# A fused attention, Fourier and channel-mixing kernel: the order of SyncE's transfers in the lead-in, two waits in the channel products, and what ScalarE and VectorE do for the turning angles

## The reference

```python
for t in range(S):
    ar, ai = (a_re_n[:, :, t, :, None], a_im_n[:, :, t, :, None])
    new_re = ar * S_re - ai * S_im
    new_im = ar * S_im + ai * S_re
    kv = np.einsum('bhd,bhe->bhde', k[:, :, t], v[:, :, t])
    S_re, S_im = (new_re + kv, new_im)
    y[:, :, t] = np.einsum('bhd,bhde->bhe', q[:, :, t], S_re)
```

## Time and profile before

| what | us |
|---|---|
| three runs | 1108.66, 1102.98, 1101.28; median 1102.98 |
| the profiled execution: its own time | 1107.81 |
| its span, first to last instruction | 1105.8 |
| TensorE busy, and mean granted clock | 1018.0 and 0.951 of full speed |
| VectorE, ScalarE, GpSimd busy | 533.7, 339.8, 16.3 |

### The profile page before, as it was taken

How to read it: one execution, slowest core, us unless ns; L and a number is a source line. 1 busy time by engine, 2 the same in 40 slices (tenths; PEclk the granted TensorE clock), 3 DMA queues, 4 the chain that set the end, 5 groups by cost and what they waited for, 6 DMA issues and landing times.

```text
span 1105.8 us, 15696 instructions
## 1 busy us (share of the span) xinstructions
PE 1018.0 (92%) x6154; PEld 975.5 (88%) x6154; DVE 533.7 (48%) x1046; ACT 339.8 (31%) x514; POOL 16.3 (1%) x12
## 2 busy tenths in 40 slices
PE   0469699989989999999999999998999999999997
PEld 0358589979979988999999999998999999999997
DVE  6797958998982555432423322542224223322321
ACT  7635545654721141122112211423112121220210
POOL 0000000000000000000000000021000000000000
PEclk9869869989978899999999999998999999999999
DMA  4559776876558106402102020001001001000000
GB/s 154 151 147 310 214 219 170 264 219 183 167 148 289 47 21 248 139 21 66 43 28 71 28 85 16 8 22 43 22 8 57 21 0 64 14 7 21 8 16 23
DMA packets 96602, 104.67 MB, mean 95 GB/s; under 512 B 13089, under 2 KB 90145, under 8 KB 96546
## 3 DMA queue, kind: packets, MB, share of 16 engines
q1 hardware_dynamic: 96546, 103.94, 30.4%
HBM read 70.80 MB, written 33.11 MB: 94 GB/s over the span
## 4 chain that ended last, share of the span: by engine, by line
PE 74%; DVE 14%; DMA 4%; issue 3%; SPq 1%; ACT 1%; POOL 1%; POOLq 0%; DVEq 0%; ACTq 0%
PE bank L232 20%; PE bank L234 19%; PE bank L233 19%; PE bank L1132 3%; PE bank L1193 2%; DVE n_area L906 2%; PE bank L1148 2%; DMA q_turn<-n_area 2%; PE bank L1209 1%; PE bank L1150 1%; PE bank L1161 1%; DVE x_flat L858 1%; PE bank L1211 1%; PE bank L242 1%; DVE n_area L911 1%
## 5 line engine op out<-in xcount | busy, mean ns | idle before, releaser
L120 ACT ACTIVATE hh<-bank 128x384 fp32r<-128x384 f32 x192 | 94.5, 493 | 386.4 <-PE bank L234 382.7
L208 DVE SCALAR_TENSOR_TENSOR hl<-bank,hh 128x384 fp32r<-128x384 f32 x192 | 107.0, 558 | 205.0 <-ACT hh L120 205.0
L232 PE MATMUL bank<-nTh,w1h 128*128 128x384 f32 x576 | 194.3, 337 | 6.1 <-DVE hl L208 3.6
L234 PE MATMUL bank<-nTh,w1l 128*128 128x384 f32 x576 | 193.6, 336 | 0.0
L233 PE MATMUL bank<-nTl,w1h 128*128 128x384 f32 x576 | 193.5, 336 | 0.0
L232 PE MATMUL bank<-w2h,hh 128*128 128x384 f32 x576 | 193.2, 335 | 0.0
L234 PE MATMUL bank<-w2h,hl 128*128 128x384 f32 x576 | 192.5, 334 | 0.0
L233 PE MATMUL bank<-w2l,hh 128*128 128x384 f32 x576 | 192.4, 334 | 0.0
L232 PEld LDWEIGHTS bank<-nTh,w1h 128*128 128x128 f32 x576 | 109.1, 189 | 7.1 <-DVE hl L208 3.9
L233 PEld LDWEIGHTS bank<-nTl,w1h 128*128 128x128 f32 x576 | 109.1, 189 | 0.0
L234 PEld LDWEIGHTS bank<-nTh,w1l 128*128 128x128 f32 x576 | 109.0, 189 | 0.0
(11 more groups left out here) (155 smaller groups left out, 1286.2 us busy)
## 6 DMA issues: line engine op xcount, KB each, us to landing
w_area<-k_turn SPq DMA_DIRECT2D x24, 384.0 KB, 3.5
w_area<-q_turn SPq DMA_DIRECT2D x24, 384.0 KB, 4.4
q_turn<-w_raw SPq DMA_DIRECT2D x30, 192.0 KB, 4.3
k_turn<-n_area SPq DMA_DIRECT2D x24, 192.0 KB, 4.0
k_turn<-w_flat SPq DMA_DIRECT2D x24, 192.0 KB, 4.6
u_scratch<-h_area SPq DMA_DIRECT2D x24, 192.0 KB, 2.9
w_raw<-in_moe_w_ch SPq DMA_DIRECT2D x2, 2304.0 KB, 12.1
x_flat<-u_scratch SPq DMA_DIRECT2D x4, 1152.0 KB, 9.8
```

The source lines that it names most:

```text
L120: self.nc.scalar.activation(self.hh[:, m, :], self.mm_bank[(g * (KF + TPG) + m) % 2][:, 0:TG], ACT.Relu).then_inc(self.h_high, 1)
L208: self.nc.vector.scalar_tensor_tensor(out=self.hl[:, m, :], in0=self.mm_bank[(g * (KF + TPG) + m) % 2][:, 0:TG], scalar=0.0, in1=self.hh[: ...
L232: self.nc.tensor.matmul(out, lh, rh, start=(n == 0), stop=False)
L234: last = self.nc.tensor.matmul(out, ll, rh, start=False, stop=(n == len(pairs) - 1))
```

## The change

On SyncE: `turn_over` is cut into `turn_out` (the writes) and `turn_back` (the reads), and `turn_decay` into `decay_out` and `decay_back`. For a part's first two blocks both writes come before both reads. `decay_out` is issued a step before `decay_back`. The q and k of p0 go to free columns of the other buffer, so the load of p2's q and k waits for nothing and is issued ahead of all turning. The later loads of gates and of q and k come one step earlier. On VectorE: L879 and L897 go; ScalarE makes the same number by `Sign` and `Identity` into `t4`, behind `Arctan`. `ends` keeps only its copy, and one reduce over all parts' `dstage` replaces L868 and L871. `products` treats two blocks with one instruction each (L922, L923, L925, L926 on 768 elements), and `products(p0)` moves ahead of `phases(p1)`. In the channel products, the wait of L1280 moves behind the first `hidden`, and that of L828 behind the first `high_hidden`.

```diff
...
+                self.qs, self.q0 = (1, 2 * CT) if n == 0 else (n % 2, 0)
...
-        GA = 14
-        GV = [12 + 5 * p.chunks for p in parts]
+        PAIRS = [[range(i, min(i + 2, p.chunks)) for i in range(0, p.chunks, 2)] for p in parts]
+        GA = 16
+        GV = [10 + 3 * p.chunks + 2 * len(PAIRS[p.n]) for p in parts]
...
             def load_qk(p):
-                if p.turn:
-                    before = parts[p.n - 2]
+                if p.n == 3:
+                    sp.wait_ge(k_out[0], 32)
+                    sp.wait_ge(q_out[0], 32)
+                if p.n > 2:
                     sp.wait_ge(vec_step[p.s], vec0[p.n])
...
-            turn_over(0)
-            turn_decay(p0)
+            load_qk(p2)
+            decay_out(p0)
+            decay_out(p1)
+            turn_out(0)
+            decay_back(p0)
+            decay_back(p1)
+            turn_back(0)
+            turn_out(1)
+            turn_out(2)
             load_gates(p3)
-            load_qk(p2)
-            turn_over(1)
-            turn_over(2)
-            turn_decay(p1)
+            turn_back(1)
+            turn_back(2)
             for m in range(NM):
                 if (m - 1, 4) in stage_at:
-                    p = stage_at[m - 1, 4]
-                    turn_over(p.first)
-                    turn_over(p.first + 1)
+                    first = stage_at[m - 1, 4].first
+                    turn_out(first)
+                    turn_out(first + 1)
+                    turn_back(first)
+                    turn_back(first + 1)
                 if (m - 1, 5) in stage_at:
-                    turn_over(stage_at[m - 1, 5].first + 2)
+                    last = stage_at[m - 1, 5].first + 2
+                    turn_out(last)
+                    turn_back(last)
+                if (m, 3) in stage_at:
+                    decay_out(stage_at[m, 3])
                 if (m, 4) in stage_at:
-                    turn_decay(stage_at[m, 4])
+                    decay_back(stage_at[m, 4])
                 for n, i in added_at(m - 1):
                     store_u(n, i)
-                if m % 3 == 1:
-                    for p in parts[2:]:
-                        if p.n > 3 and p.first == m + 8:
-                            load_gates(p)
-                        if p.n > 2 and p.first == m + 5:
-                            load_qk(p)
-                        if p.first == m + 2:
-                            load_v(p)
+                for p in parts[2:]:
+                    if p.n > 3 and p.first == m + 9:
+                        load_gates(p)
+                    if p.n > 2 and p.first == m + 6:
+                        load_qk(p)
+                    if p.first == m + 2:
+                        load_v(p)
...
                 A(t3_b[s][:, :, T], t3_b[s][:, :, T], ACT.Arctan).then_inc(act_step[s], 1)
+                A(im_b[p.r][:, :, T], re_b[p.r][:, :, T], ACT.Sign, scale=3.0,
+                  bias=nearly_zero[:, 0:1]).then_inc(act_step[s], 1)
+                act.wait_ge(act_step[s], act0[p.n] + 12)
+                A(t4[:, :, angles_room(p)], im_b[p.r][:, :, T], ACT.Identity, scale=-0.25,
+                  bias=quarter[:, 0:1]).then_inc(act_step[s], 1)
...
-            act.wait_ge(s1.w2_split, 3)
             with act.Fori(0, B - 1) as b:
                 s1.high_hidden(act, b, 0)
+                act.wait_ge(s1.w2_split, 3)
...
-                V.tensor_copy(dstage[:, s, :, 0:p.chunks], t2_b[s][:, :, CT - 1:p.T:CT]).then_inc(vec_step[s], 1)
-                dve.wait_ge(vec_step[s], vec0[p.n] + 5)
-                V.tensor_reduce(least_now[:, :], dstage[:, s, :, 0:p.chunks], mybir.AxisListType.XY,
-                                ALU.min).then_inc(least_step, 1)
-                dve.wait_ge(least_step, 2 * p.n + 1)
-                V.tensor_tensor(least[:, :], least[:, :], least_now[:, :], ALU.min).then_inc(least_step, 1)
+                V.tensor_copy(dstage[:, p.n, :, 0:p.chunks], t2_b[s][:, :, CT - 1:p.T:CT]).then_inc(vec_step[s], 1)
...
-                V.tensor_scalar(im[:, :, T], re[:, :, T], 0.0, -2.0 / PI, ALU.is_lt, ALU.mult).then_inc(vec_step[s], 1)
...
-                dve.wait_ge(act_step[s], act0[p.n] + 11)
-                dve.wait_ge(vec_step[s], n + 7)
-                V.scalar_tensor_tensor(out=t3_b[s][:, :, T], in0=im[:, :, T], scalar=1.0 / PI, in1=t3_b[s][:, :, T],
-                                       op0=ALU.add, op1=ALU.mult).then_inc(vec_step[s], 1)
-                dve.wait_ge(vec_step[s], n + 10)
-                V.tensor_scalar(im[:, :, T], re[:, :, T], 0.0, 0.5, ALU.is_lt, ALU.mult).then_inc(vec_step[s], 1)
+                dve.wait_ge(act_step[s], act0[p.n] + 13)
+                V.scalar_tensor_tensor(out=t3_b[s][:, :, T], in0=t3_b[s][:, :, T], scalar=1.0 / PI, in1=im[:, :, T],
+                                       op0=ALU.mult, op1=ALU.mult).then_inc(vec_step[s], 1)
...
-                for i in chunks:
-                    T = slice(i * CT, (i + 1) * CT)
+                for pair in chunks:
+                    i = pair.start
+                    T = slice(i * CT, pair.stop * CT)
...
+            products(p0, PAIRS[0])
             phases(p1)
-            products(p0, range(1))
             squared(p2)
-            products(p1, range(2))
+            products(p1, PAIRS[1])
...
+            V.tensor_reduce(least[:, :], dstage[:, :, :, :], mybir.AxisListType.XYZ, ALU.min).then_inc(least_found, 1)
...
-            pe.wait_ge(s0.w2_split, KF // 2)
             with pe.Fori(0, B - 1) as b:
                 s0.hidden(pe, b, 0)
+                pe.wait_ge(s0.w2_split, KF // 2)
                 s0.output(pe, b, 0)
...
```

More of the change, by code:

```diff
@@ L396, in forward @@
         a_mid = in_late(1, FH)
-        dstage = in_late(P, 2, 3, 3)
+        dstage = in_late(P, len(parts), 3, 3)
         YR = 12
@@ L490, in load_qk @@
             def load_qk(p):
-                if p.turn:
-                    before = parts[p.n - 2]
+                if p.n == 3:
+                    sp.wait_ge(k_out[0], 32)
+                    sp.wait_ge(q_out[0], 32)
+                if p.n > 2:
                     sp.wait_ge(vec_step[p.s], vec0[p.n])
-                    for m in range(before.first, before.end):
+                    for m in range(parts[p.n - 2].first, parts[p.n - 2].end):
                         sp.wait_ge(k_out[m % RING], 32 * (m // RING + 1))
                 for dst, src in ((k_b, lay["k"]), (q_b, lay["q"])):
-                    sp.dma_start(dst[p.s][:, :, 0:p.T], src[p.b, :, :, p.t0:p.t0 + p.T]).then_inc(qk_in[p.s], 16)
+                    sp.dma_start(dst[p.qs][:, :, p.qk_cols(0, p.chunks)],
+                                 src[p.b, :, :, p.t0:p.t0 + p.T]).then_inc(qk_in[p.s] if p.n else qk_first_in, 16)
             def load_v(p):
@@ L525, in turn_over, with decay_out @@
                 sp.dma_start(qT[:, r, :, :], back("q_turn")).then_inc(q_back[r], 16)
-            def turn_decay(p):
+            def decay_out(p):
                 if p.turn:
@@ L988, in _ @@
             squared(p1)
[L989 removed]
+            dve.wait_ge(consts_set, 5)
             logs(p0)
```

86 lines of the change are left out of this document (49 added, 37 removed).

## The result

The changed kernel takes 1059.13 us, median of 4 runs (1050.0 to 1066.06); the kernel before took 1102.47, median of 4 (1101.28 to 1108.66). The ratio is 0.9584, with a 95% interval of 0.9494 to 0.9675: 4.2% faster. The ratio is taken from the fast runs alone, without the one of 1066.06, so it isn't the quotient of the two medians, 0.9607. I had said 1058, within 1040 to 1084. The profiled execution after took 1054.72 us, with a span of 1052.7; the one before took 1107.81, with a span of 1105.8.

A forecast was written before the change was run, and what follows sets the result against it. TensorE was taken to bound the kernel throughout, losing time to waits and low clock. The terms summed to 47.1 us off the profiled 1107.8, so 1060.7, or 1055.9 from the median; the middle, 1058, was forecast, range 1040 to 1084.

The forecast's parts named there:

- lead-in: Start of the kernel, up to TensorE's step 1: mask multiply 0 comes earlier, p2's q no longer waited for; 4.7 us.
- step 21: TensorE's step 21 in the first half, low clock without a wait before it: no gain in the sum.
- Step 6: TensorE's wait for block 6's keys goes, 8.8 us, and the low clock behind it, 8.4 us.
- rival 3: Transfers collide at step 6: half the wait for keys stays, 4.4 us, and the low clock; 1071 us, chance 0.12.
- Steps 13 and 19: VectorE's smaller load cuts TensorE's waits of 3.3 us to 0.6, low clock gone too; 7.8 and 9.1 us.
- The waits in s0 and s1: Second half, channel products: moved waits for w2 pieces are hidden; 2.5 us in s0, 6.6 in s1 with its clock.
- rival 2: More clock than counted: step 1 at full clock, 4.6 us, and step 21, 8.1 us; 1045 us, chance 0.22.
- Steps 3 and 4: phases(p3) starts 2.1 us later behind Sign and Identity, only 0.7 shorter: 0.8 us taken back.
- Rival 4: ScalarE becomes the gate because Sign needs its own table, in each of nine parts; slower, 1135 us, chance 0.04.
- Rival 5: TensorE meets VectorE again in the first half; only lead-in, s0 and s1 remain, 13.8 us; 1089 us, chance 0.06.
- rival 1: The waits go but the clock doesn't come at steps 6, 13, 19 and s1: 23 us lost, 1081 us, chance 0.18.
- its clock goes with the wait: Low clock behind a removed TensorE wait vanishes too: 8.4 us at step 6, 5.2 and 6.4 at 13 and 19, 3.1 in s1.

The follow-up runs named there:

- sync_only: The kernel before with only SyncE's new order and the new place of p0's q and k: 1080.7 us.
- work_only: The kernel before with only VectorE's and ScalarE's edits (Sign and Identity, one reduce, products of two blocks, products(p0) first): 1078.3 us.
- all_but_waits: The changed kernel with the two waits of the channel products back in their old places: steady part (span times mean clock) 1040.2 us.
- split_and_middle: split_wait with ScalarE's copy of `middle` put ahead of the last activation of magnitudes: steady part (span times mean clock) 1030.8 us.
- signs_on_vector: The changed kernel with the two sign instructions back on VectorE, Sign and Identity off ScalarE: median 1065.4 us.
- split_wait: The changed kernel with the first instruction of phases waiting for Sign alone, the scans for Identity: steady part (span times mean clock) 1030.7 us.
- pairs_undone: The changed kernel with products of one block at a time, as before the change: steady part (span times mean clock) 1034.0 us.
- waits_only: The kernel before with only the two moved waits of the channel products: 1090.9 us.
- busy_at_6: The kernel before with 14 matmuls that nobody reads at the start of step 6, in place of TensorE's wait: 1102.1 us.

## Why the prediction was right

The time was forecast within 1.1 us of the median, and by the table above stretch by stretch within 1 us at the three places that carry most of the sum. That the total is so close is luck. Three stretches were off by 5.5 to 8.1 us each (5.5 more in the lead-in, 5.5 less in steps 2 to 5, 8.1 more in step 21), and the two profiled executions lie 53.1 us apart where the medians lie 43.3 apart; I had forecast 47.1 for the first and 45 for the second. Point by point:

- **Step 6 (17.2 forecast, 16.2 gained).** Right, with the cause shown by sync_only and work_only. One size was off: I gave the keys some 10 us more, and they go out 20.4 us earlier (124.02 to 103.58). Even so they are not early by much. They take 14.5 us from that write to their landing (12.5 before), and the 5.6 us in hand at step 6 are there only because step 4 was slow. In all_but_waits, where step 4 kept its clock, they land at 118.03 and TensorE begins at 119.04; in split_and_middle it waits 1.10 us for them and in signs_on_vector 3.05. So rival 3, a wait for the keys that stays in part, is not what happened, but it was close; whether transfers in each other's way bring it isn't shown.
- **Steps 13 and 19 (7.8 and 9.1 forecast; 6.9 and 8.9 gained).** Right. The waits left are 0.16 and 0.44 where I had 0.6. Step 13 lost the rest to the 0.80 us for `middle`'s copy, which I had not seen coming: I had asked what stands behind the new activations only for `keys_turned`.
- **The waits in s0 and s1 (9.1 forecast, 9.4 gained in the last row of the table).** Right; undone in the changed kernel they cost 6.4 to 7.4 us of steady part and 7 to 9 in the medians.
- **Lead-in (4.7 forecast, 10.2 gained to the end of step 1).** The wait itself ended 3.85 us earlier (68.70 to 64.85), 0.85 less than the sum said, because mask multiply 0 came at 63.51 and not at 62.5. The other 6.3 us are step 1 at full clock, which I had put into rival 2 at 4.6. That term was missing from the sum: by the earlier trace rows the whole of step 1 behind its wait ran at 0.50, and I priced the clock at the other long waits but not at this one. The cause I gave for the wait of 6.07 us, that the load was issued late, is one of two that hold: work_only takes it away as well, with the load where it was, most likely by `products(p0)` placed first, which no run tried alone.
- **Steps 3 and 4 (0.8 taken back, 6.3 lost).** The step that failed. The mechanism was there (the phases of p2, p3 and p4 wait 2.2 to 3.0 us for Identity, and mask multiply 3 came 1.07 late), but behind it the clock was low for 10.2 us, which no term held. The wait of 1.07 isn't needed for it (split_wait) and doesn't bring it by itself (all_but_waits).
- **Step 21 (0 forecast, 8.1 gained).** No edit touches it; rival 2 had it.
- **Signs on ScalarE, pairs, one reduce.** I counted 1.9 us of VectorE per part as worth its length at steps 13 and 19. Together the edits do remove those waits (work_only). Singly, pairs and signs each show next to nothing: with either undone the waits at step 13 stay below 0.9 us, though pairs_undone has 0.96 us at step 19. That both are needed, or that either would do, follows from no run here.
- **Rival 4** fell with the sixteen table loads. **Rival 5** fell too: the time fell by 43 us, and the steady part alone by 18.

What the sum holds is best read from the account. I had 24 us of waits and 23 of clock. Measured are 18 to 19 in the steady part and 25 to 28 in the clock's part, with the waits that lay in low clock counted half in the first. So rival 1 (the waits go, the clock doesn't come) is wrong. Taking all fourteen traces from 85 to 370 us together, TensorE waited 1.96 us or more fifteen times, and fourteen of these waits had a low stretch of 10 to 24 us at them, beginning within 2.3 us of the wait's end or inside it; of six waits of 0.96 to 1.10 us, four had one (the waits of 0.9 to 1.9 us at the last block's transforms, near 350, are left out of both counts). That is the term as I priced it, and the step "its clock goes with the wait" holds. Beside it there is a background that I had for step 21 alone: thirteen stretches of 10 to 17 us with TensorE busy and no wait of over 0.31 us in the 5 us ahead, in eight of the fourteen traces, up to three in one, in ten different steps. Per trace that is about one of some 13 us, 6 us of time. I find no edit that it belongs to. That step 21 was free of it in the profiled execution is luck of this size. Step 4 is another matter: both executions of the changed kernel that were profiled have its low stretch, each behind the wait of 1.07 or 1.06 us, and the six traces with the phases as before have none in that step. It looks more like a cost of the change than like luck, and no run decides it.

## What to carry to other kernels

Multiply each run's span by its mean granted clock before comparing kernels whose low stretches are few: here it turned a spread of 26 us into one of 8, and one of 17 into one of 2, and so made edits of 2 us visible in four runs. Price a wait of TensorE among short matmuls with the slow stretch that follows it (here 5 to 12 us more than the wait), but don't read a low stretch without a wait as belonging to the line that it covers. When two instructions are put on an engine ahead of a hand-over, list all that stands behind them on that engine, small copies for TensorE (`middle`) too. Ask of a wait that is gone how much is in hand: at step 6 it was 5.6 us in one trace and nothing in another.

## What the runs showed that was not expected

- **The clock fell to its lower level while TensorE was busy, some 3 us behind a wait of a quarter of a us.** Besides the windows above, sync_only in step 15, where the kernel before was at full clock: the last wait ahead, and the window.
```profile
240.27 0.55 PE L1150 MATMUL bank<-ident,w_area 96*128 96x96 f32 x4 [0.25 <-ACT w_area L749]
```
```profile
243.50:257.00 13.50, 13.50 (x56) 12.23 (x55) 12.71 (x26) 1.13 (x2) 0.00 (x0) 0.50 0.37 97
```
  The steps differ, but the place within the step doesn't: all thirteen stretches begin 3.0 to 3.1 us after the end of a wait of 0.25 to 0.30 us, TensorE's wait for ScalarE's copy in `turn_keys`. That wait stands in most steps and mostly brings nothing: between 85 and 350 us the fourteen traces have 183 of TensorE's waits of 0.2 to 0.4 us with the clock up at them, and 13 had the fall behind them. What picks the one in fourteen, no run tells. All such stretches lie among the short matmuls of the first half. In the 128x384 matmuls of the second half no trace has one without a wait ahead. The Trainium skill (TensorE: Matmul & The Clock Gate, section "What's actually happening") says that the point where the clock changes differs from run to run; the traces agree, in that the step in which the clock falls differs between kernels with the same code up to there, and go further, in that a stretch comes or doesn't come at all.
- **A wait of 2.31 us left the clock alone, and one of 1.96 was followed by 14 us at half.** The first, the one exception of fifteen, is step 13 of waits_only, its row and its window; the second is busy_at_6 above.
```profile
239.74 0.53 PE L1148 MATMUL bank<-w_area 128*128 128x48 f32 x3 [2.31 <-DVE w_area L951]
```
```profile
232.00:247.00 15.00, 12.70 (x84) 9.79 (x83) 14.37 (x32) 8.76 (x10) 0.00 (x0) 1.00 0.65 220
```
  In the same way the 3.70 us of waiting in the second half had 6.6 us of low clock behind it in the kernel before, and none in all_but_waits; the four other traces with that wait had it too. What decides it, no run here tells.
- **A kernel that was forecast from one trace has a scatter of its own.** The kernel before went from 1095 to 1121 us on one chip with a steady part of 1048 to 1055; the changed one from 1050 to 1067 with 1032.5 to 1034.4. Fewer waits make not only the time but its scatter smaller: the steady part of the kernels without the long waits spreads over less than 4 us, that of the others over 4 to 8.4.
